# Queries without zero blocks: score and state products of 48 rows, two heads on two row tiles

## The chip, the cores and the metric

The kernel runs on one core of one Trainium2 chip. The metric is the device time of one execution in microseconds; the median of the runs counts. All arithmetic that matters here is float32.

## What is computed

Three layers in a row: a linear-attention recurrence, a soft mixture of experts, and an MLP with a squared ReLU. Only the first is touched. For 4 images (batch), 8 heads, 768 tokens and head size 48:

```python
for t in range(S):
    kt, vt, rt = (k[:, :, t], v[:, :, t], r[:, :, t])
    cur = np.einsum('bhd,bhe->bhde', u[None] * kt, vt)
    y[:, :, t] = np.einsum('bhd,bhde->bhe', rt, state + cur)
    state = w[None, :, :, None] * state + np.einsum('bhd,bhe->bhde', kt, vt)
```

`_moe_ref` then mixes the 3072 tokens of width 384 into 32 slots, sends each slot through one of 8 experts and mixes back, and `_moe2_ref` is `relu(x @ w_in)**2 @ w_out`.

## The kernel before, in words

The recurrence is done in six chunks of 128 tokens, and each chunk in four head pairs: 24 units, numbered n = 4 c + hp. A unit covers all four images b and both heads of its pair. The two heads stand on partitions 0 to 47 and 64 to 111 (`HEAD_ROWS`; `PAIR` is 112 partitions).

Each engine has its own program, in an order written by hand, and semaphores tie them together. One unit takes:

- SyncE (`load_unit`, line 314): loads `rk` (r and k with tokens last), once the queries of two units before are done, then `rkv` (r, k and v with tokens first) and a piece of the experts' weights.
- VectorE (`chunk`, in this order): `scale` multiplies k and r by powers of the decay, into `keys` (line 638) and `queries` (line 644). Then it waits for the diagonal of the unit before (`diag_done`). `advance` updates the state of two units before (line 680; in the first chunk a copy, line 676). `mask_scores` (line 667) copies the previous unit's scores from PSUM over the diagonal, where the mask says so. `sum_bonus` (line 662) sums `ruk`; `scale_n` (line 653) makes `keys_n`.
- GpSimd: `products` makes `ruk` = r u k in two steps (lines 402 and 405); `diagonal` (line 413) writes the bonus on the diagonal of `scores`, zero elsewhere, for the unit before. GpSimd runs one unit ahead with `ruk`.
- TensorE: `unit_scores` (line 865), then `unit_output` of the unit before, then `unit_state` (line 904).
- ScalarE copies the output and the state's increment out of PSUM.

`queries` has a block of zeros for each head: of an image's 256 columns the first 128 hold head 0 on partitions 0 to 47 with zeros below, the other 128 hold head 1 on partitions 64 to 111 with zeros above. One matmul of 112 rows and 256 columns then gives both heads' scores without mixing them, and the state product (line 887) of one head may take all 112 rows of the pair's state. GpSimd clears the four `queries` buffers once, at the start (line 395); VectorE fills the two blocks with one product each.

`unit_output` writes `y_ps`, one PSUM bank: for each image, two state products (not in the first chunk), then two products of masked scores and values (line 890), head 0 to partitions 0 to 47, head 1 to partitions 64 to 111. So they all work on two column tiles, with 112 or 128 rows.

The second unit of every chunk but the first (and the end) also brings the previous chunk's output into token order and forms its logits: `pair_logits` (line 839), a group of transposes (`turn_x`, line 847) after each image's scores, and `token_logits` (line 854). That is done between the unit's scores and the output of the unit before.

After the last unit come the experts and the MLP, whose weights are loaded as the recurrence frees their room.

Of the kernel before, what the change touches and what calls it, by code (L numbers as in the profile page):

```python
# [54 lines left out]
def program(nc, rk_t, rkv_n, w_t, u, phi, w1, w2, w_in, w_out, out):  # L55
# [32 lines left out]
    queries = [place(f"queries{i}", [P, B, 2, P]) for i in range(4)]  # L88
# [3 lines left out]
    scores = [place(f"scores{i}", [P, B, 2, P]) for i in range(2)]  # L92
# [5 lines left out]
    bonus = [place(f"bonus{i}", [P, B, 2]) for i in range(2)]  # L98
# [17 lines left out]
    assert place.end <= loads_end and queries_at == room_at + 4 * KD * FE and 4 * KE * DM <= 4 * (HP - 1) * B * 2 * P  # L116
# [49 lines left out]
    with stack:  # L166
# [30 lines left out]
        q_cleared = sem("q_cleared")  # L197
# [179 lines left out]
        def _(pool):  # L377
# [16 lines left out]
            for i in range(HP):  # L394
                nc.gpsimd.memset(queries[i][:, :, :, :], 0.0).then_inc(q_cleared, 1)
# [13 lines left out]
            def diagonal(m, hp):  # L409
# [4 lines left out]
                    scores[hp % 2][:, :, :, :].rearrange("p b h t -> p (b h) t"),  # L414
                    ident[:, :].unsqueeze(1).broadcast_to([P, 2 * B, P]),
                    bonus[hp % 2][:, :, :].rearrange("p b h -> p (b h)").unsqueeze(2).broadcast_to([P, 2 * B, P]),
# [175 lines left out]
        def _(ve):  # L592
# [40 lines left out]
            def scale(c, hp):  # L633
# [7 lines left out]
                if isinstance(c, int) and c == 0:  # L641
                    ve.wait_ge(q_cleared, hp + 1)
                for half, rows in enumerate(HEAD_ROWS):
                    last = nc.vector.tensor_tensor(queries[hp][rows, :, half], rk[hp % 2][rows, 0],  # L644
                                                   q_pow[rows, hp].unsqueeze(1).broadcast_to([D, B, P]), ALU.mult)
                last.then_inc(qk_done, 1)
# [10 lines left out]
            def sum_bonus(c, hp):  # L657
# [4 lines left out]
                nc.vector.reduce_sum(bonus[hp % 2][:, :, :], ruk[hp % 2][:, :, :].rearrange("p b (h d) -> p b h d", d=D),  # L662
                                     AX.X).then_inc(bonus_done, 1)

            def mask_scores(hp):

                nc.vector.copy_predicated(scores[hp % 2][:, :, :, :].rearrange("p b h t -> p (b h) t"),  # L667
# [165 lines left out]
        def _(pe):  # L833
# [24 lines left out]
            def unit_scores(c, hp, with_x):  # L858
# [5 lines left out]
                for b in range(B):  # L864
                    last = nc.tensor.matmul(score_ps[hp % 2][:, 2 * P * b:2 * P * (b + 1)], keys[hp % 2][0:PAIR, b],  # L865
                                            queries[hp][0:PAIR, b].rearrange("p h t -> p (h t)"), start=True, stop=True)
# [9 lines left out]
            def unit_output(m, c, hp):  # L876
# [6 lines left out]
                for b in range(B):  # L883
                    cols = slice(P * b, P * (b + 1))
                    if carried:
                        for half in range(2):
# [38 lines left out]
            chunk(0, True)  # L925
            pe.wait_ge(params_in, 3 * 16)
            pe.wait_ge(const_step, FOLD)
            chunk(1, False)
            with pe.Fori(2, CH) as c:
                chunk(c, False)  # L930

# [217 lines left out]
```

## Time and profile before

| | us |
|---|---|
| median of 3 runs | 467.32 |
| lowest, highest | 465.28, 467.35 |
| span of the profiled execution, first to last instruction | 464.3 |
| busy in it: TensorE, VectorE, ScalarE, GpSimd | 405.0, 331.9, 174.4, 153.1 |

No time of the profiled execution other than its span is shown; the median is 3.0 us above the span. The busy times are over the whole span, in which the recurrence is the first 176 us or so and the MLP the last 230. The page's chain of waits has 43% of the span in the MLP's output matmuls, which the change does not touch, and for the recurrence the diagonal on GpSimd (8%), the mask (4%) and the queries (4%). A row of the timeline merges neighbours of one line and operation ("x8"); in brackets stand the engine's idle time before it and what ended it. A float32 matmul leaves two records, so eight records are four matmuls.

### The profile page before, as it was taken

The page shows a single profiled execution, that of the slowest core. Times are in us where ns is not written, and L with a number is a line of the kernel's source. Part 1 is how long each engine was busy: PE and PEld are TensorE (multiplying, and loading weights), DVE is VectorE, ACT ScalarE, POOL GpSimd, SP SyncE. Part 2 cuts the span into 40 slices and gives each one's busy share as a digit, 9 for nine tenths or more (in the row PEclk, how much of TensorE's full clock was granted, in tenths as well). Part 3 has the DMA queues.
Part 4 walks back from the last instruction along what each step waited for, and adds up shares of the span by engine and source line. Part 5 has one row for each costly group of instructions (what it writes and reads, how often), then busy time and mean ns, then how long its engine had stood idle before and what let it go on. Part 6 is the DMA issues. An engine that isn't in the chain of part 4 may idle for free.

```text
span 464.3 us, 8783 instructions
## 1 busy us (share of the span) xinstructions
PE 405.0 (87%) x3096; PEld 349.0 (75%) x3096; DVE 331.9 (71%) x439; ACT 174.4 (38%) x312; POOL 153.1 (33%) x111
## 2 busy tenths in 40 slices
PE   0856968778787889999679999999999999999997
PEld 0544857657676766235279999999999999999997
DVE  8599999999999994611596565565556556556553
ACT  2011313123031314012535555555555555555552
POOL 6578878898888850110550000000000000000000
PEclk9957999999998989899889999999999999999999
DMA  6966667667666769999600010001001001001001
GB/s 174 243 195 193 202 206 218 183 201 231 194 196 203 225 238 316 373 373 403 212 0 1 1 68 2 1 1 68 0 0 68 0 0 68 0 0 68 1 0 68
DMA packets 31844, 60.30 MB, mean 130 GB/s; under 512 B 2640, under 2 KB 25296, under 8 KB 31440
## 3 DMA queue, kind: packets, MB, share of 16 engines
q1 hardware_dynamic: 31824, 60.02, 40.9%
q8 instruction: 13, 0.21, 0.2%
q14 instruction: 7, 0.06, 0.1%
HBM read 55.30 MB, written 4.72 MB: 129 GB/s over the span
## 4 chain that ended last, share of the span: by engine, by line
PE 61%; DVE 14%; POOL 10%; issue 5%; DVEq 1%; ACT 1%; POOLq 0%; ACTq 0%
PE out_ps L1081 43%; POOL scores L413 8%; PE h_ps L1059 5%; DVE scores L667 4%; DVE queries L644 4%; PE wide L997 3%; PE wide L1022 2%; PE score_ps L865 2%; DVE bonus L662 1%; DVE state L680 1%; PE y_ps L890 1%; POOL ruk L402 1%; POOL ruk L405 1%; PE wide L948 1%; DVE keys L638 1%
## 5 line engine op out<-in xcount | busy, mean ns | idle before, releaser
L1081 PE MATMUL out_ps<-w_hi,act_hi 128*128 128x384 f32 x384 | 130.5, 340 | 5.2 <-DVE act_lo L819 4.0
L1081 PE MATMUL out_ps<-w_hi,act_lo 128*128 128x384 f32 x384 | 131.0, 341 | 0.0
L1081 PE MATMUL out_ps<-w_lo,act_hi 128*128 128x384 f32 x384 | 130.5, 340 | 0.0
L814 DVE TENSOR_TENSOR act<-relu_h 128x512 f32<-128x512 f32 x96 | 68.2, 711 | 78.3 <-ACT relu_h L576 78.3
L576 ACT ACTIVATE relu_h<-h_ps 128x512 f32<-128x512 f32 x96 | 57.3, 597 | 100.6 <-PE h_ps L1059 97.9
L865 PE MATMUL score_ps<-queries,keys 112*128 112x256 f32 x192 | 60.5, 454 | 29.7 <-DVE queries L644 29.7
L413 POOL TENSOR_TENSOR scores<-ident,bonus 128x1024 f32<-128x1024 f32 x24 | 74.4, 3101 | 23.2 <-DVE bonus L662 23.2
L1081 PEld LDWEIGHTS out_ps<-w_hi,act_hi 128*128 128x128 f32 x384 | 72.7, 189 | 6.2 <-ACT act_hi L579 3.3
L1081 PEld LDWEIGHTS out_ps<-w_lo,act_hi 128*128 128x128 f32 x384 | 72.9, 190 | 3.8
L1081 PEld LDWEIGHTS out_ps<-w_hi,act_lo 128*128 128x128 f32 x384 | 72.5, 189 | 0.0
L819 DVE TENSOR_TENSOR act_lo<-act,act_hi 128x512 fp32r<-128x512 f32 x96 | 68.4, 713 | 4.6 <-ACT act_hi L579 1.0
L865 PEld LDWEIGHTS score_ps<-queries,keys 112*128 112x128 f32 x192 | 39.3, 222 | 41.8 <-DVE queries L644 24.1
L644 DVE TENSOR_TENSOR queries<-rk,q_pow 48x512 f32<-48x512 f32 x48 | 67.4, 1405 | 0.3
L579 ACT ACTIVATE act_hi<-relu_h 128x512 fp32r<-128x512 f32 x96 | 60.9, 634 | 3.9
L474 ACT ACTIVATE x_t<-y_ps 112x512 f32<-112x512 f32 x24 | 14.3, 597 | 111.2 <-PE y_ps L890 111.2
L890 PE MATMUL y_ps<-scores,rkv 128*48 128x128 f32 x384 | 38.0, 286 | 1.8 <-DVE scores L667 1.8
L1059 PE MATMUL h_ps<-mix_t,gin 128*128 (+1 forms) x96 | 38.0, 398 | 0.0
L887 PE MATMUL y_ps<-queries,state 112*48 112x128 f32 x320 | 32.6, 278 | 4.3 <-DVE scores L667 4.1
L667 DVE COPY_PREDICATED scores<-mask,score_ps 128x1024 f32<-128x1024 uint32 x24 | 32.0, 1333 | 4.8 <-POOL scores L413 4.8
L402 POOL TENSOR_TENSOR ruk<-rkv 128x384 f32<-128x384 f32 x24 | 31.0, 1291 | 10.8 <-DMA rkv<-in_rkv_n 8.5
L890 PEld LDWEIGHTS y_ps<-scores,rkv 128*48 128x48 f32 x384 | 24.6, 129 | 4.3 <-DVE scores L667 2.9
L887 PEld LDWEIGHTS y_ps<-queries,state 112*48 112x48 f32 x320 | 18.6, 123 | 10.8 <-issue 7.5
(145 smaller groups left out, 369.1 us busy)
## 6 DMA issues: line engine op xcount, KB each, us to landing
rkv<-in_rkv_n SPq DMA_DIRECT2D x24, 576.0 KB, 4.6
rk<-in_rk_t SPq DMA_DIRECT2D x48, 192.0 KB, 3.2
w_sb<-in_w SPq DMA_DIRECT2D x24, 384.0 KB, 5.1
w_room<-in_w SPq DMA_DIRECT2D x4, 1536.0 KB, 11.1
out_dram<-y_sb SPq DMA_DIRECT2D x5, 768.0 KB, 3.5
w_x<-in_w SPq DMA_DIRECT2D x2, 1536.0 KB, 14.0
w_w<-in_w SPq DMA_DIRECT2D x4, 768.0 KB, 11.5
w_in_sb<-in_w_in SPq DMA_DIRECT2D x3, 1024.0 KB, 13.0
```

The costliest lines, as they stand in the source:

```text
L413: nc.gpsimd.tensor_tensor(scores[hp % 2][:, :, :, :].rearrange("p b h t -> p (b h) t"), ident[:, :].unsqueeze(1).broadcast_to([P, 2 * B, P ...
L576: nc.scalar.activation(relu_h[f % 2][:, :], h_ps[f % 4][:, :], ACT.Relu).then_inc(relu_done, 1)
L579: nc.scalar.activation(act_hi[f % 4][:, :], relu_h[f % 2][:, :], ACT.Square).then_inc(act_hi_done, 1)
L644: last = nc.vector.tensor_tensor(queries[hp][rows, :, half], rk[hp % 2][rows, 0], q_pow[rows, hp].unsqueeze(1).broadcast_to([D, B, P]), AL ...
L667: nc.vector.copy_predicated(scores[hp % 2][:, :, :, :].rearrange("p b h t -> p (b h) t"), mask[:, :].unsqueeze(1).broadcast_to([P, 2 * B, P]),
L814: nc.vector.tensor_tensor(act[f % 2][:, :], relu_h[f % 2][:, :], relu_h[f % 2][:, :], ALU.mult).then_inc(act_done, 1)
L819: nc.vector.tensor_tensor(act_lo[f % 4][:, :], act[f % 2][:, :], act_hi[f % 4][:, :].bitcast(F32), ALU.subtract).then_inc(act_lo_done, 1)
L865: last = nc.tensor.matmul(score_ps[hp % 2][:, 2 * P * b:2 * P * (b + 1)], keys[hp % 2][0:PAIR, b], queries[hp][0:PAIR, b].rearrange("p h t ...
L887: nc.tensor.matmul(y_ps[SECOND * half:SECOND * half + D, cols], state[0:PAIR, hp, b], queries[hp][0:PAIR, b, half], start=True, stop=False)
L890: last = nc.tensor.matmul(y_ps[SECOND * half:SECOND * half + D, cols], rkv[hp][:, 2, b, D * half:D * (half + 1)], scores[hp % 2][:, b, hal ...
L1059: nc.tensor.matmul(h_ps[f % 4][:, :], gin[:, P * f:P * (f + 1)], mix_t[:, bass.ds(g * B, B), :], start=True, stop=True).then_inc(h_mm, 1)
L1081: last = nc.tensor.matmul(out_ps[t][:, 0:DM], a[f % 4][:, tok], w[:, f], start=(f == 0 and i == 0), stop=(f == NF - 1 and i == 2))
```

## The change

`queries` becomes one block: 112 partitions, 4 images, 128 tokens, and VectorE fills it with one product. GpSimd's clearing and its semaphore go. The scores of an image become two matmuls of 48 rows and 128 columns, one for each head: head 0 on rows 0 to 47, head 1 on rows 64 to 111, each into a PSUM bank of its own. The state products take the 48 rows of their head. `scores` and `bonus` are laid out by head first. TensorE's loop over the chunks is written out. Buffers elsewhere stay where they are (a gap of 8 KB a partition keeps them there).

```diff
@@ -85,17 +85,18 @@
-    queries = [place(f"queries{i}", [P, B, 2, P]) for i in range(4)]
+    cursor[0] += 4 * (KE * DM - 2 * B * P)
+    queries = [place(f"queries{i}", [P, B, P]) for i in range(4)]
...
-    scores = [place(f"scores{i}", [P, B, 2, P]) for i in range(2)]
+    scores = [place(f"scores{i}", [P, 2, B, P]) for i in range(2)]
...
-    bonus = [place(f"bonus{i}", [P, B, 2]) for i in range(2)]
+    bonus = [place(f"bonus{i}", [P, 2, B]) for i in range(2)]
...
@@ -391,8 +391,6 @@
-            for i in range(HP):
-                nc.gpsimd.memset(queries[i][:, :, :, :], 0.0).then_inc(q_cleared, 1)
...
@@ -638,12 +636,9 @@
                 wait(ve, y_done, n - 3)
-                if isinstance(c, int) and c == 0:
-                    ve.wait_ge(q_cleared, hp + 1)
-                for half, rows in enumerate(HEAD_ROWS):
-                    last = nc.vector.tensor_tensor(queries[hp][rows, :, half], rk[hp % 2][rows, 0],
-                                                   q_pow[rows, hp].unsqueeze(1).broadcast_to([D, B, P]), ALU.mult)
-                last.then_inc(qk_done, 1)
+                nc.vector.tensor_tensor(queries[hp][0:PAIR], rk[hp % 2][0:PAIR, 0],
+                                        q_pow[0:PAIR, hp].unsqueeze(1).broadcast_to([PAIR, B, P]),
+                                        ALU.mult).then_inc(qk_done, 1)
...
@@ -862,8 +857,10 @@
                 for b in range(B):
-                    last = nc.tensor.matmul(score_ps[hp % 2][:, 2 * P * b:2 * P * (b + 1)], keys[hp % 2][0:PAIR, b],
-                                            queries[hp][0:PAIR, b].rearrange("p h t -> p (h t)"), start=True, stop=True)
+                    for half, rows in enumerate(HEAD_ROWS):
+                        at = BANK * half + P * b
+                        last = nc.tensor.matmul(score_ps[hp % 2][:, at:at + P], keys[hp % 2][rows, b],
+                                                queries[hp][rows, b], start=True, stop=True)
...
@@ -883,13 +880,13 @@
                     if carried:
-                        for half in range(2):
-                            nc.tensor.matmul(y_ps[SECOND * half:SECOND * half + D, cols], state[0:PAIR, hp, b],
-                                             queries[hp][0:PAIR, b, half], start=True, stop=False)
+                        for rows in HEAD_ROWS:
+                            nc.tensor.matmul(y_ps[rows, cols], state[rows, hp, b], queries[hp][rows, b],
+                                             start=True, stop=False)
                     for half in range(2):
                         last = nc.tensor.matmul(y_ps[SECOND * half:SECOND * half + D, cols],
                                                 rkv[hp][:, 2, b, D * half:D * (half + 1)],
-                                                scores[hp % 2][:, b, half], start=not carried, stop=True)
+                                                scores[hp % 2][:, half, b], start=not carried, stop=True)
...
@@ -925,8 +922,7 @@
-            chunk(1, False)
-            with pe.Fori(2, CH) as c:
+            for c in range(1, CH):
                 chunk(c, False)
```

On VectorE, one unit of the second chunk, in program order (names are buffers, numbers their copies). Before:

```order
L638 TENSOR_TENSOR keys_58<-rk_56,k_pow 112x512
L644 TENSOR_TENSOR queries_62<-rk_56,q_pow 48x4x128 x2
L680 SCALAR_TENSOR_TENSOR state<-state,w_88,state_in_74 112x192
L667 COPY_PREDICATED scores_73<-mask,score_ps 128x1024
L662 TENSOR_REDUCE bonus_79<-ruk_68 128x8
L653 TENSOR_TENSOR keys_n_70<-rkv_66,kn_pow 128x384
```

Now:

```order
L636 TENSOR_TENSOR keys_58<-rk_56,k_pow 112x512
L639 TENSOR_TENSOR queries_62<-rk_56,q_pow 112x512
L675 SCALAR_TENSOR_TENSOR state<-state,w_88,state_in_74 112x192
L662 COPY_PREDICATED scores_73<-mask,score_ps 128x1024
L657 TENSOR_REDUCE bonus_79<-ruk_68 128x4x2
L648 TENSOR_TENSOR keys_n_70<-rkv_66,kn_pow 128x384
```

One queries product stands where two stood; the order of the rest is the same.

On TensorE, the unit that also turns the previous chunk's output, from its pair logits into the output of the unit before. Before:

```order
L839 MATMUL lg_ps<-x_t,phi_sb 32x512 x4
L865 MATMUL score_ps<-queries_61,keys_59 128x256
L847 MATMUL x_ps<-ident,x_t 128x112 x4
L865 MATMUL score_ps<-queries_61,keys_59 128x256
L847 MATMUL aux_ps<-ident,x_t 128x112 x4
L865 MATMUL score_ps<-queries_61,keys_59 128x256
L847 MATMUL x_ps<-ident,x_t 128x112 x4
L865 MATMUL score_ps<-queries_61,keys_59 128x256
L847 MATMUL aux_ps<-ident,x_t 128x112 x4
L854 MATMUL lg_ps<-fold_50,logits_t 128x128 x4
L887 MATMUL y_ps<-queries_60,state 48x128 x2
L890 MATMUL y_ps<-scores_72,rkv_64 48x128 x2
```

Now:

```order
L834 MATMUL lg_ps<-x_t,phi_sb 32x512 x4
L862 MATMUL score_ps<-queries_61,keys_59 128x128 x2
L842 MATMUL x_ps<-ident,x_t 128x112 x4
L862 MATMUL score_ps<-queries_61,keys_59 128x128 x2
L842 MATMUL aux_ps<-ident,x_t 128x112 x4
L862 MATMUL score_ps<-queries_61,keys_59 128x128 x2
L842 MATMUL x_ps<-ident,x_t 128x112 x4
L862 MATMUL score_ps<-queries_61,keys_59 128x128 x2
L842 MATMUL aux_ps<-ident,x_t 128x112 x4
L849 MATMUL lg_ps<-fold_50,logits_t 128x128 x4
L884 MATMUL y_ps<-queries_60,state 48x128 x2
L887 MATMUL y_ps<-scores_72,rkv_64 48x128 x2
```

Each image's scores are two matmuls of 128 columns in place of one of 256; nothing changed places. The state and output pairs of line 887 and 890 (now 884 and 887) alternate through all four images, as before.

## Rows read from the trace of the kernel before

**Rows 1.** The page's forty equal slices of the span: busy tenths.
```profile
DVE  8599999999999994611596565565556556556553
```

**Rows 2.** Views of source lines 644 and 413: duration ns min/median/max, first and last start.
```profile
L644 DVE TENSOR_TENSOR queries<-rk,q_pow x48: 672/692/2374, 10.2 to 169.3; 48x512 f32<-48x512 f32 x48
...
L413 POOL TENSOR_TENSOR scores<-ident,bonus x24: 1894/3333/3352, 18.7 to 172.2; 128x1024 f32<-128x1024 f32 x24
```

**Rows 3.** Timeline of one unit: start us, us, engine, line, operation, operands, count.
```profile
105.21 0.55 DVE L662 TENSOR_REDUCE bonus<-ruk 128x8 f32<-128x384 f32 x1
...
105.66 0.56 DVE L653 TENSOR_TENSOR keys_n<-rkv,kn_pow 128x384 f32<-128x384 f32 x1
...
105.83 3.33 POOL L413 TENSOR_TENSOR scores<-ident,bonus 128x1024 f32<-128x1024 f32 x1 [0.92 <-DVE bonus L662]
...
106.13 0.69 DVE L638 TENSOR_TENSOR keys<-rk,k_pow 112x512 f32<-112x512 f32 x1
...
106.73 2.98 DVE L644 TENSOR_TENSOR queries<-rk,q_pow 48x512 f32<-48x512 f32 x2
...
109.46 1.11 POOL L402 TENSOR_TENSOR ruk<-rkv 128x384 f32<-128x384 f32 x1 [0.30 <-DMA rkv<-in_rkv_n]
...
109.74 1.04 DVE L680 SCALAR_TENSOR_TENSOR state<-state,w,state_in 112x192 f32<-112x192 f32 x1
...
110.71 1.33 DVE L667 COPY_PREDICATED scores<-mask,score_ps 128x1024 f32<-128x1024 uint32 x1
...
111.93 0.54 DVE L662 TENSOR_REDUCE bonus<-ruk 128x8 f32<-128x384 f32 x1
```

**Rows 4.** Timeline of GpSimd, 10 to 180 us: the third and the twenty-third of 24 diagonals.
```profile
31.52 3.33 POOL L413 TENSOR_TENSOR scores<-ident,bonus 128x1024 f32<-128x1024 f32 x1 [1.87 <-DVE bonus L662]
...
165.95 2.21 POOL L413 TENSOR_TENSOR scores<-ident,bonus 128x1024 f32<-128x1024 f32 x1
```

**Rows 5.** Timeline of TensorE in a heavy unit; lastly the whole kernel's row of line 854.
```profile
98.80 0.43 PE L887 MATMUL y_ps<-queries,state 112*48 112x128 f32 x4 [0.44 <-DVE scores L667]
...
101.45 1.06 PE L839 MATMUL lg_ps<-x_t,phi_sb 112*32 112x512 f32 x8 [0.33 <-ACT x_t L474]
...
103.02 0.70 PE L865 MATMUL score_ps<-queries,keys 112*128 112x256 f32 x2 [0.50 <-DVE queries L644]
...
106.43 1.07 PE L854 MATMUL lg_ps<-fold,logits_t 128*128 128x128 f32 x8
...
107.43 0.43 PE L887 MATMUL y_ps<-queries,state 112*48 112x128 f32 x4
...
107.69 0.39 PE L890 MATMUL y_ps<-scores,rkv 128*48 128x128 f32 x4
...
109.01 0.39 PE L890 MATMUL y_ps<-scores,rkv 128*48 128x128 f32 x4
...
L854 PE MATMUL lg_ps<-fold,logits_t 128*128 128x128 f32 x48 | 6.4, 277 | 0.0
```

**Rows 6.** Timeline of VectorE near the end: a state update that waits for nothing.
```profile
163.63 0.42 DVE L680 SCALAR_TENSOR_TENSOR state<-state,w,state_in 112x192 f32<-112x192 f32 x1
```

**Rows 7.** Timeline of the recurrence's start, on GpSimd and VectorE.
```profile
11.30 1.15 POOL L402 TENSOR_TENSOR ruk<-rkv 128x384 f32<-128x384 f32 x1 [2.27 <-DMA phi_sb<-in_phi]
...
25.00 3.78 DVE L644 TENSOR_TENSOR queries<-rk,q_pow 48x512 f32<-48x512 f32 x2
...
27.24 0.99 POOL L402 TENSOR_TENSOR ruk<-rkv 128x384 f32<-128x384 f32 x1 [0.41 <-DMA rkv<-in_rkv_n]
```

**Rows 8.** Stretches (busy by engine, granted clock, DMA); scores at either clock.
```profile
24.50:31.52 7.02, 2.68 (x6) 2.19 (x7) 6.98 (x7) 0.30 (x1) 4.66 (x5) 0.50 0.55 152
...
112.55:119.37 6.82, 4.48 (x64) 3.80 (x61) 6.77 (x8) 0.82 (x2) 5.75 (x4) 1.00 0.68 201
...
28.84 3.78 PE L865 MATMUL score_ps<-queries,keys 112*128 112x256 f32 x8 [4.41 <-DVE queries L644]
...
109.77 1.99 PE L865 MATMUL score_ps<-queries,keys 112*128 112x256 f32 x8
```

More of the change, by code:

```diff
@@ L115, in program @@
     assert 2 * B * P == FE
-    assert place.end <= loads_end and queries_at == room_at + 4 * KD * FE and 4 * KE * DM <= 4 * (HP - 1) * B * 2 * P
+    assert place.end <= loads_end and queries_at == room_at + 4 * KD * FE
     experts_at = place.end
@@ L196, in program @@
         ps_cleared = sem("ps_cleared")
-        q_cleared = sem("q_cleared")
         const_step = sem("const_step")
@@ L413, in diagonal @@
                 nc.gpsimd.tensor_tensor(
-                    scores[hp % 2][:, :, :, :].rearrange("p b h t -> p (b h) t"),
+                    scores[hp % 2][:, :, :, :].rearrange("p h b t -> p (h b) t"),
                     ident[:, :].unsqueeze(1).broadcast_to([P, 2 * B, P]),
-                    bonus[hp % 2][:, :, :].rearrange("p b h -> p (b h)").unsqueeze(2).broadcast_to([P, 2 * B, P]),
+                    bonus[hp % 2][:, :, :].rearrange("p h b -> p (h b)").unsqueeze(2).broadcast_to([P, 2 * B, P]),
                     ALU.mult).then_inc(diag_done, 1)
@@ L661, in sum_bonus @@
                 wait(ve, diag_done, n - 1)
-                nc.vector.reduce_sum(bonus[hp % 2][:, :, :], ruk[hp % 2][:, :, :].rearrange("p b (h d) -> p b h d", d=D),
+                nc.vector.reduce_sum(bonus[hp % 2][:, :, :].rearrange("p h b -> p b h"), ruk[hp % 2][:, :, :].rearrange("p b (h d) -> p b h d", d=D),
                                      AX.X).then_inc(bonus_done, 1)
             def mask_scores(hp):
-                nc.vector.copy_predicated(scores[hp % 2][:, :, :, :].rearrange("p b h t -> p (b h) t"),
+                nc.vector.copy_predicated(scores[hp % 2][:, :, :, :].rearrange("p h b t -> p (h b) t"),
                                           mask[:, :].unsqueeze(1).broadcast_to([P, 2 * B, P]),
```

## The prediction

> **What bounds the kernel now.** The forty slices of the page come first: VectorE is at nine tenths through the first fifteen slices, the recurrence, and only there [rows 1]. The change touches nothing behind it except through the moment at which the recurrence ends. Next, the summary of single source lines: a queries product takes 0.67 us at least and 2.37 at most, the diagonal product on GpSimd 1.89 at least and mostly 3.33 [rows 2]. Two engines that at times stretch each other. The timeline of one unit shows how [rows 3]. The diagonal starts at 105.83 but ends 1.44 us later than an undisturbed one would, and it gets going just where the first queries product ends (106.73 + 0.67 = 107.40; 107.40 to its end 109.16 is 1.76). The pair of queries products takes 2.98: the second half runs only when the diagonal has ended, and ends 0.55 behind it, at 109.71. Then the first `ruk` product takes its turn (until 110.57, 0.86 behind 109.71), and the state update waits for that, 1.04 us where an undisturbed one took 0.42 [rows 6]. So products with two operands in SBUF take turns with GpSimd's, one at a time, and VectorE is never idle. One unit, bonus to bonus, is 111.93 - 105.21 = 6.72 us, and the twenty units between two diagonals far apart average (165.95 - 31.52) / 20 = 6.72 [rows 4]. The last view is TensorE's timeline in the one unit of four that also turns the previous chunk's output (I call it heavy) [rows 5].
>
> **The base.** The profiled execution spans 464.3 us; the median of the three times is 467.3, so 3.0 lie around the span or between executions. The change is summed on the profiled execution and applied to the median.
>
> **VectorE's edit.** One of two queries products goes; the one left has 112 partitions and as many elements in each, like the keys product, which takes 0.69 [rows 3], so the width is free. What that is worth is not 24 times the mean of 1.4, most of which is waiting. In the unit of rows 3 the order before the diagonal stays: bonus, keys_n, keys, one queries product, 2.19 us from the bonus's start; then the diagonal's 1.76. Behind it stood the second queries product for 0.55. Now nothing stands there, and the next to ask is the `ruk` product, which GpSimd starts as soon as the diagonal ends; the state update cannot start sooner than 0.58 us behind it (109.74 - 109.16). So `ruk` goes first: about 0.09 to begin (its undisturbed 0.99 [rows 7] less the 0.86, less the little by which it overlaps the diagonal's end), 0.86, then 0.22 of the state update (its end 110.78 less 110.57), then 1.15 to the next bonus. Sum: 2.19 + 1.76 + 0.09 + 0.86 + 0.22 + 1.15 = 6.27; gain 0.45 a unit, **9.0 us over twenty units**. The ends: nothing, if the freed turn is only waited out elsewhere; 1.0 a unit if the state update slips in ahead of `ruk`. I take 0.45, from the order in which rows 3 show the starts. At the beginning, the unit at 25.00 has both queries products blocked, 3.78 in all, one by the diagonal and one by a `ruk` [rows 7]: between 0.7 and 1.4 less, I take 1.0. The four memsets are worth nothing: GpSimd waits 2.27 us for a DMA before its first product anyway [rows 7]. The layouts of `scores` and `bonus` keep their elements: nothing. On SyncE the loads that wait for the queries go out some 2.3 us sooner, past nothing else; that helps no one, since the next keys come a unit later.
>
> **TensorE's edit, plain part.** The scores of one image were one product of 256 columns; now two of 128 columns on two row tiles. No row here has two row tiles. The nearest are two column tiles, the pairs of the output: between 107.69 and 109.01 six groups of four records take 0.22 each, 0.055 a record, where records of 128 columns on the whole array come every (1.07 - 0.28) / 7 = 0.113 [rows 5]. So pairs on column tiles overlap. If row tiles do too, the scores of a unit lose 4 x 0.22 = 0.9 us; if not, nothing. I take 0.9. The state products were already pairs on column tiles, and stay 0.22 an image.
>
> Writing out the loop over the chunks removes a branch at the first unit of a chunk, a light one, where TensorE has idle time to hide it, and adds instructions to fetch: nothing both ways; in the heavy unit, without that cover, neither falls.
>
> **TensorE's edit, the switches.** The state products now use 64 rows and 48 columns, the output products beside them all 128 rows, and they alternate image by image: seven changes of tile shape inside each unit's output. Rows 5 show what a change of shape (there, of the columns alone) costs: after eight records from 106.43 the next should start at 107.34, and starts at 107.43; the next group follows after 0.26 in place of 0.22. Together 0.13. So the output of a unit grows by 7 x 0.13 = 0.9. In the heavy unit the scores (64 rows) alternate with the turned output (128 rows, 128 columns of weights): seven more, each about 0.10 plus one record's 0.11 for weights that can no longer be loaded ahead, an estimate from the same rows, 0.21: 1.5. The ends are nothing (shapes that differ in rows alone need no pause) and twice this.
>
> **Does that reach the end?** In a light unit no: its TensorE work is 4.48 of 6.82 us [rows 8], it loses 0.9 and gains 0.9. In the heavy unit, yes. From the start of one unit's output (98.80) to the end of the next one's (109.01 + 0.39 = 109.40) TensorE needs 10.6, and the state update that waits for it starts at 109.74: 0.34 to spare. After: 10.6 + 0.9 + 0.9 (two outputs) + 1.5 - 0.9 (scores) - 0.5 (the wait for queries between 102.51 and 103.02, which come sooner) = 12.5. Allowed were 10.94; two shorter periods take 0.9, the mask that opens the first output comes 0.46 sooner behind the diagonal, and the update may start some 0.15 later before it delays anything: 10.65. **Late by 1.85, five times, 9.2 us.** The last output of all has no other work beside it, and adds 0.9.
>
> **Sum.** -9.0 - 1.0 + 9.2 + 0.9 = +0.1: VectorE's gain is given back on TensorE. Forecast 467, no change that can be told (under 0.5%, 2.3 us).
>
> **Rivals.**
> *No pause between row shapes.* TensorE then needs 10.6 - 0.9 - 0.5 = 9.2 of 10.65 and never binds: -9.0 - 1.0, 457. For it: what rows 5 show are changes of columns. Against: the pause there is the same kind of event, and the rows of the array are in use in both shapes.
> The Trainium skill, "TensorEngine Tiling (Array Packing)", Overview, says that changing the tiling mode drains the engine, rows or columns alike, without a price; by it, the forecast's side of this question is the right one.
>
> *The two heads' state products do not overlap.* Both write `y_ps`, one PSUM bank, from two row tiles, where today two column tiles write it. Taken one after the other they add 4 x 0.22 = 0.9 to each unit's output, 1.8 to the heavy chain, 9 us in five, 0.9 at the tail: 477, slower. It decides from the point at which a pair costs 0.06 more than now. Nothing in the profile speaks for or against row tiles sharing a bank; for column tiles they overlap.
> The Trainium skill, same page, Restrictions and Gotchas, says that row tiles cannot access one PSUM bank at the same time; by it the time would be this rival's. No run here shows it yet.
>
> *TensorE's clock.* In the stretch 24.50 to 31.52 the granted clock is 0.50 (1.2 GHz), and the scores take 3.78 for eight records, 1.99 at 1.00 [rows 8]. A light unit after the change has fewer columns to stream. At 1.2 GHz its 4.5 us would be some 8.5, 2 us over the period: two such units are felt, five make 477. Against: the light unit of rows 8 is granted 1.00 though it idles a third of the time.
>
> *The port goes strictly to who asked first.* The diagonal, started during keys_n, would then run ahead of keys and queries, and the `ruk` products would fall between these; the state update would come last: bonus 0.45, keys_n 0.55, diagonal 1.76, then keys, `ruk`, queries, `ruk` (2 x 0.55 + 2 x 0.86), 0.22, 1.15, 6.95 a unit, 472. Rows 3 speak against it: keys and the first queries product went ahead of a waiting diagonal.
> The Trainium skill, "SBUF — State Buffer", Who interferes with whom, has the pair of ports as an exclusive lock for whoever issues first; the trace agrees on the lock (0.67 against 2.37), not on the order.
>
> *The state update ahead of `ruk`*, and no pause on TensorE: 5.7 a unit, 446.
>
> **Chances.** Forecast (both halves nearly cancel, 463 to 471) 0.37; no pause 0.25; no overlap 0.15; clock 0.12; state ahead 0.05; first asked 0.04; something else 0.02. Of the forecast's 0.37 I count 0.24 within 0.5%, the rest half to each side. Faster: 0.25 + 0.05 + 0.07 = 0.37; slower: 0.15 + 0.12 + 0.03 + 0.06 + 0.01 = 0.37; same 0.26. The range 455 to 478 takes in the first four cases with their ends; the likeliest alone would be 463 to 471.
>
> **What would show it.** Right: light units of about 6.27 from diagonal to diagonal, the unit after a heavy one near 8.1; queries a single row of 0.7; `ruk` directly behind the diagonal and the state update at 1 us or more; output records with a gap of about 0.13 at each state-to-output change; the idle time before the state update put down to TensorE's `y_ps`. Wrong: the unit after a heavy one no longer than the others (no pause); state records in pairs 0.1 apart rather than together (no overlap); a granted clock of 0.50 inside the recurrence beyond its first 50 us; a diagonal of 1.9 to 2.4 with keys behind it (order of the port).

## The result and the profile after

The changed kernel takes 480.22 us in the median of four executions (476.86 to 492.12), the kernel before 466.43 beside it: a ratio of **1.027, 95% interval 1.020 to 1.033, slower**. The forecast was no change, 467, in a range of 455 to 478: wrong, and outside the range. (Ratios here leave out executions over 1.5% above the fastest of their kernel, medians and profiles don't: where a kernel's times scatter, the two differ by up to 1%.)

The page of the changed kernel first: VectorE's slices, then TensorE's granted clock by slice.
```profile
DVE  7586564654636517370198556556556556556553
PEclk9996958869659569999978999999999999999999
```
The same row of the kernel before:
```profile
PEclk9957999999998989899889999999999999999999
```
VectorE, at nine tenths before [rows 1], is at three to eight, mostly four to six: it no longer bounds the recurrence. Between the fourth and the fifteenth slice TensorE's clock, at eight tenths and more from the fifth slice on before, dips to five and six tenths again and again.

The profiled execution spans 480.3, 16.0 more than before. The third diagonal starts at 29.26 and the twenty-third at 182.22 (31.52 and 165.95 before [rows 4]): the start gains 2.3, the twenty units lose 18.5 (152.96 against 134.43), the unit behind them gains 0.7, and all that follows loses 0.4. So the question is about the twenty units alone. Stretches of the changed kernel, each from one diagonal to the next (length, busy us of PE, PEld, DVE, ACT, POOL, granted clock, DMA share, GB/s):
```profile
85.33:91.67 6.34, 4.42 (x68) 2.87 (x68) 4.50 (x7) 0.82 (x2) 5.29 (x3) 1.00 0.82 259
91.67:97.90 6.23, 6.23 (x60) 4.12 (x56) 3.72 (x7) 0.93 (x2) 5.23 (x4) 0.51 0.64 180
97.90:105.34 7.44, 7.38 (x60) 3.02 (x56) 3.77 (x7) 0.93 (x2) 5.29 (x4) 0.50 0.65 192
105.34:115.53 10.19, 9.68 (x114) 6.79 (x112) 3.77 (x7) 3.67 (x8) 5.30 (x4) 0.99 0.47 146
115.53:121.89 6.36, 4.43 (x68) 2.87 (x68) 4.51 (x7) 0.82 (x2) 5.29 (x4) 1.00 0.81 248
121.89:128.10 6.21, 6.21 (x62) 4.16 (x60) 4.05 (x7) 0.93 (x2) 5.22 (x4) 0.55 0.66 202
128.10:135.43 7.33, 7.27 (x58) 2.94 (x56) 4.00 (x7) 0.93 (x2) 5.29 (x3) 0.50 0.58 177
135.43:148.77 13.34, 12.81 (x110) 9.24 (x112) 3.78 (x7) 3.65 (x8) 5.30 (x4) 0.71 0.32 92
```
A pattern of four: a light unit at full clock (6.34 and 6.36; 6.27 was forecast), one of the same length near half clock (1.2 GHz), one of 7.3 to 7.4 at half clock, in which TensorE is busy nearly throughout, and the stretch of the heavy unit (the heavy stretch from here on), 10.2 or 13.3. The five heavy stretches are 7.34, 9.22, 10.19, 13.34 and 13.55 long. At 13.34 TensorE is busy for 12.81 at a mean clock of 0.71.

Who waits for it shows in the summary of VectorE's lines, the state update of the changed kernel over the twenty units (17 records; in the first chunk it is a copy, on another line):
```profile
L675 DVE SCALAR_TENSOR_TENSOR state<-state,w,state_in 112x192 f32<-112x192 f32 x17 | 12.8, 750 | 64.7 <-PE y_ps L887 55.2 <-POOL scores L411 9.5
```
and of the kernel before:
```profile
L680 DVE SCALAR_TENSOR_TENSOR state<-state,w,state_in 112x192 f32<-112x192 f32 x17 | 16.6, 977 | 1.4 <-PE y_ps L890 0.9
```
VectorE idles 55.2 us for TensorE's output where it idled 0.9.

The timeline of TensorE in the changed kernel has an output at full clock, and the scores alternating with the turned output at half clock:
```profile
110.20 0.42 PE L884 MATMUL y_ps<-queries,state 48*48 48x128 f32 x4
110.55 0.43 PE L887 MATMUL y_ps<-scores,rkv 128*48 128x128 f32 x4
110.91 0.42 PE L884 MATMUL y_ps<-queries,state 48*48 48x128 f32 x4
...
135.33 0.80 PE L862 MATMUL score_ps<-queries,keys 48*128 48x128 f32 x4
136.06 1.00 PE L842 MATMUL x_ps<-ident,x_t 112*128 112x112 f32 x4
137.00 0.80 PE L862 MATMUL score_ps<-queries,keys 48*128 48x128 f32 x4
...
146.62 1.16 PE L862 MATMUL score_ps<-queries,keys 48*128 48x128 f32 x16
```
Groups of four records, state and output by turns, come every 0.355 us where they came every 0.22 [rows 5]: 0.135 for each change of shape. The scores of a whole unit take 1.16 at full clock, 1.99 before [rows 8]: two row tiles do run side by side (here each writes its own PSUM bank). An image of the heavy unit takes 1.67 at half clock (137.00 - 135.33).

VectorE and GpSimd in a light unit of the changed kernel, by the timeline:
```profile
115.53 3.35 POOL L411 TENSOR_TENSOR scores<-ident,bonus 128x1024 f32<-128x1024 f32 x1 [4.81 <-DVE bonus L657]
118.83 0.99 POOL L400 TENSOR_TENSOR ruk<-rkv 128x384 f32<-128x384 f32 x1
...
116.43 0.69 DVE L639 TENSOR_TENSOR queries<-rk,q_pow 112x512 f32<-112x512 f32 x1
...
118.96 1.08 DVE L675 SCALAR_TENSOR_TENSOR state<-state,w,state_in 112x192 f32<-112x192 f32 x1 [1.85 <-POOL scores L411]
```
One queries product of 0.69, the diagonal ending 1.76 behind it, then `ruk`, then the state update: the order and lengths that the prediction worked out of [rows 3].

### The profile page after: what moved, and what is told of

Its sections match the earlier page's. It is cut to its first block, busy times and chain, and to the rows that moved or that the text cites. A ratio compares the mean times of both kernels' runs of the same rounds, so it can differ in the third digit from the quotient of the medians.

```text
span 480.3 us, 9086 instructions
## 1 busy us (share of the span) xinstructions
PE 432.5 (90%) x3288; PEld 347.6 (72%) x3288; DVE 276.4 (58%) x415; ACT 175.6 (37%) x312; POOL 144.2 (30%) x107
## 4 chain that ended last, share of the span: by engine, by line
PE 71%; POOL 5%; issue 5%; DVE 4%; DMA 3%; ACT 1%; SPq 1%; DVEq 1%; POOLq 0%; ACTq 0%
PE out_ps L1077 43%; PE y_ps L884 5%; PE y_ps L887 5%; POOL scores L411 5%; PE h_ps L1055 5%; PE score_ps L862 3%; DMA w_w<-in_w 3%; DVE scores L662 2%; PE lg_ps L834 2%; PE x_ps L842 1%; PE aux_ps L842 1%; PE lg_ps L849 1%; PE wide L993 1%; SPq L355 1%; PE wide L944 1%
## 5 line engine op out<-in xcount | busy, mean ns | idle before, releaser
L1077 PE MATMUL out_ps<-w_hi,act_hi 128*128 128x384 f32 x384 | 131.9, 343 | 4.0 <-DVE act_lo L814 2.4
L411 POOL TENSOR_TENSOR scores<-ident,bonus 128x1024 f32<-128x1024 f32 x24 | 76.2, 3176 | 48.9 <-DVE bonus L657 48.9
L887 PE MATMUL y_ps<-scores,rkv 128*48 128x128 f32 x384 | 48.2, 352 | 8.6 <-DVE scores L662 8.4
L884 PE MATMUL y_ps<-queries,state 48*48 48x128 f32 x320 | 40.2, 335 | 12.5 <-DVE scores L662 12.5
L675 DVE SCALAR_TENSOR_TENSOR state<-state,w,state_in 112x192 f32<-112x192 f32 x18 | 13.2, 732 | 66.6 <-PE y_ps L887 55.2
L862 PE MATMUL score_ps<-queries,keys 48*128 48x128 f32 x384 | 41.7, 358 | 3.8 <-DVE queries L639 3.8
L862 PEld LDWEIGHTS score_ps<-queries,keys 48*128 48x128 f32 x384 | 32.6, 243 | 15.6 <-issue 8.8
L887 PEld LDWEIGHTS y_ps<-scores,rkv 128*48 128x48 f32 x384 | 21.5, 147 | 29.1 <-issue 19.4
L884 PEld LDWEIGHTS y_ps<-queries,state 48*48 48x48 f32 x320 | 15.2, 135 | 30.7 <-DVE scores L662 15.2
L400 POOL TENSOR_TENSOR ruk<-rkv 128x384 f32<-128x384 f32 x24 | 24.0, 1000 | 7.3 <-DMA rkv<-in_rkv_n 4.9
```

The source lines that it names most:

```text
L400: nc.gpsimd.tensor_tensor(ruk[hp % 2][:, :, :], rkv[hp][:, 0], rkv[hp][:, 1], ALU.mult).then_inc(rk_prod_done, 1)
L411: nc.gpsimd.tensor_tensor(scores[hp % 2][:, :, :, :].rearrange("p h b t -> p (h b) t"), ident[:, :].unsqueeze(1).broadcast_to([P, 2 * B, P ...
L862: last = nc.tensor.matmul(score_ps[hp % 2][:, at:at + P], keys[hp % 2][rows, b], queries[hp][rows, b], start=True, stop=True)
L884: nc.tensor.matmul(y_ps[rows, cols], state[rows, hp, b], queries[hp][rows, b], start=True, stop=False)
L887: last = nc.tensor.matmul(y_ps[SECOND * half:SECOND * half + D, cols], rkv[hp][:, 2, b, D * half:D * (half + 1)], scores[hp % 2][:, half, ...
L1077: last = nc.tensor.matmul(out_ps[t][:, 0:DM], a[f % 4][:, tok], w[:, f], start=(f == 0 and i == 0), stop=(f == NF - 1 and i == 2))
```

## The experiments

Two theories. *Pauses*: the changes of tile shape make TensorE's chain around the heavy unit too long. *Clock*: with the shorter scores TensorE's clock falls, and that alone decides. The runs are called e1 to e13. All ratios are against the kernel before, run on the same chip.

### Fewer changes of shape

e1, the scores of the heavy unit ahead of all transposes:
```diff
-                    if b == B - 1:
-                        last.then_inc(score_done, 1)
-                    if with_x:
+                last.then_inc(score_done, 1)
+                if with_x:
+                    for b in range(B):
```


> The changed kernel with one thing else: in the heavy unit the eight scores products stand together ahead of the transposes, so that 7 of the 8 changes of tile shape there go. Theory 1 (the pauses at shape changes make TensorE's chain in the heavy unit too long, and the lateness is multiplied where its granted clock falls): each pause with the weights not loaded ahead is about 0.12 us (0.955 against 0.83 an image), 4 images, 0.5 to 1.5 us a heavy unit, five units, partly at half clock: 3 to 9 us less than the changed kernel, 472 to 477. Theory 2 (the granted clock alone decides, pauses are a side matter): 478 to 482, and the clock still 0.50 in the third unit of a chunk. Against both: the state update's first transposes come later in this order, which may cost the 1 us that the scores now stand in front of them; then 480 to 484.

Measured: 484.94, ratio 1.039 (1.033 to 1.045). Both theories missed the time, and the third range, 480 to 484, missed it by a little. The clock was at 0.50 to 0.56 in the third units, as the second theory has it, and at 0.69 to 0.78 in four of five heavy stretches, where the change had two such. What makes it slower than the change stays open.

e2, the state product second and first by turns:
```diff
+                    state_first = b % 2 == 1
+                    if carried and state_first:
+                        from_state()
                     for half in range(2):
                         last = nc.tensor.matmul(y_ps[SECOND * half:SECOND * half + D, cols],
...
+                    if carried and not state_first:
+                        last = from_state()
```


> The changed kernel with one thing else: in every unit's output the state product comes second and first by turns (output, state, state, output, output, state, state, output), so 4 changes of tile shape in place of 7. Theory 1: 3 pauses of 0.135 us less, 0.4 us in each of two outputs of the chain over a heavy unit, 0.8 by five, 4 us, up to 6 where the clock is at half: 474 to 476. Theory 2: less time in the output but the same columns, so the clock does as before: 478 to 481.

Measured: 470.38 in the median of ten executions from 464.51 to 480.34, ratio 1.003 (0.999 to 1.007): 10 us less than the change, more than pauses at full clock explain. Its output has eight state records in a row:
```profile
112.29 0.64 PE L886 MATMUL y_ps<-queries,state 48*48 48x128 f32 x8
112.86 0.64 PE L893 MATMUL y_ps<-scores,rkv 128*48 128x128 f32 x8
```
Four records and a change of shape took 0.355; eight take 0.57, so the second four add 0.22, as pairs on column tiles do. One after the other they would add four times 0.113 [rows 5], 0.45. The two heads' state products, on two row tiles, overlap in one PSUM bank.

e3, both:

> The changed kernel with both orders at once (scores together in the heavy unit, state products second and first by turns). Theory 1: the gains add up, 2.0 to 2.7 us a heavy unit and five of them, 10 to 14 us: 466 to 470, the unit after a heavy one 7 to 8 us where the clock is full. Theory 2: 478 to 482, or no better than the better of the two alone, with units of 10 to 13 us at a clock of 0.7 as they are now.

Measured: 466.03, ratio 0.996 (0.992 to 1.000). Its stretches:
```profile
75.29:82.06 6.77, 5.82 (x84) 4.52 (x84) 4.20 (x7) 1.97 (x5) 5.34 (x3) 1.00 0.89 249
...
94.60:100.93 6.33, 6.27 (x61) 3.75 (x60) 3.80 (x7) 1.22 (x3) 5.32 (x4) 0.58 0.73 211
100.93:109.57 8.64, 7.87 (x108) 6.25 (x106) 3.73 (x7) 3.15 (x8) 5.29 (x3) 1.00 0.51 173
```
The heavy stretch is 6.77 where the clock ahead of it was full, 8.64 behind a unit at 0.58: the clock matters. That the pauses do too is seen against e4, below: 7.87 with all of them, at full clock.

### The clock by itself

e4, the light units' scores done twice:
```diff
-                    for half, rows in enumerate(HEAD_ROWS):
+                    for half, rows in list(enumerate(HEAD_ROWS)) * (1 if with_x else 2):
```


> The changed kernel with the scores products of the three light units of a chunk done twice (the second time into the same place): TensorE has 1.16 us more to do in a unit, about as much as before the change, while the heavy units are as changed. Theory 2 (the clock falls because light units keep TensorE less busy): the granted clock stays at 1.00 in the recurrence, the slow heavy units of 13 us go, and the time falls to 467 to 473 in spite of the added work. Theory 1: the added work lies in light units with idle time; 480 to 484 and a clock that falls as before.

Measured: 466.80, ratio 0.999 (0.995 to 1.003): *more* work on TensorE took 13 us off the changed kernel, pauses unchanged. The mean granted clock of the profiled execution is 0.982, the change's 0.908. Its stretches, and of the last one the start of the output ahead of the heavy unit's scores and the end of the one behind them:
```profile
96.09:102.38 6.29, 6.24 (x62) 3.07 (x62) 4.45 (x7) 1.52 (x3) 5.31 (x3) 0.73 0.76 231
102.38:111.44 9.06, 9.06 (x117) 6.82 (x116) 3.78 (x7) 3.06 (x7) 5.29 (x3) 1.00 0.48 145
...
117.81:123.99 6.18, 5.16 (x82) 3.64 (x80) 4.08 (x7) 0.82 (x2) 5.22 (x3) 1.00 0.59 172
123.99:130.31 6.32, 5.98 (x72) 3.38 (x72) 4.47 (x7) 1.98 (x5) 5.32 (x3) 1.00 0.88 272
130.31:138.18 7.87, 7.87 (x107) 5.90 (x106) 3.77 (x7) 2.50 (x6) 5.30 (x3) 1.00 0.48 137
```
```profile
123.53 0.42 PE L884 MATMUL y_ps<-queries,state 48*48 48x128 f32 x4 [1.02 <-DVE scores L662]
135.33 0.43 PE L887 MATMUL y_ps<-scores,rkv 128*48 128x128 f32 x4
```
Where the clock is full, light units are 6.2 to 6.4, the heavy stretch is 7.87, and TensorE's chain around the heavy unit takes 12.2 us (123.53 to 135.76): the forecast's picture (6.27, 8.1 and 12.5), and the forecast's time, 467. One light unit at 0.73 makes the next heavy stretch 9.06. The five heavy stretches (7.43, 7.85, 9.06, 7.87, 9.03) are 9.9 over five of 6.27, where the forecast has 9.2. That the two sums meet so closely is in part luck: two of the five come behind a unit at 0.73, and the first, one of whose two outputs has no state products, is shorter.

### VectorE's edit and the pauses, each alone

e5, in the kernel before, one queries product:
```diff
-                for half, rows in enumerate(HEAD_ROWS):
+                for half, rows in list(enumerate(HEAD_ROWS))[:1]:
```


> The kernel before with the first of its two queries products alone: the second head's block of the queries stays zero, so the second head's scores and state products are left out of the result, while TensorE's instructions, shapes and columns are those of before. Theory (VectorE's share of the change is worth 0.45 us a unit and some 2 us at the start, and is lost on TensorE alone): units of 6.27 us, heavy ones 6.3 to 6.7, the granted clock as before, 454 to 458. Rival (TensorE binds the unit of before as closely as VectorE, so that there was nothing to gain): 464 to 467.

Measured: 456.94, ratio 0.980 (0.976 to 0.983). Two of its stretches, the first the heavy one:
```profile
97.33:103.63 6.30, 6.11 (x78) 5.32 (x78) 4.20 (x7) 2.02 (x5) 5.31 (x3) 1.00 0.73 222
103.63:109.97 6.34, 4.41 (x64) 3.79 (x61) 4.49 (x7) 0.82 (x2) 5.28 (x3) 1.00 0.76 219
```
The twenty units (28.66 to 153.86) average 6.26. VectorE's gain is real, and TensorE as it was allowed it.

e6, the changed kernel with two queries products of 48 partitions:
```diff
-                nc.vector.tensor_tensor(queries[hp][0:PAIR], rk[hp % 2][0:PAIR, 0],
...
+                for rows in HEAD_ROWS:
+                    last = nc.vector.tensor_tensor(queries[hp][rows], rk[hp % 2][rows, 0],
```


> The changed kernel with VectorE's edit undone in time: the queries product in two halves of 48 partitions, as before, TensorE as changed. Theory (light units are bound by VectorE, the unit behind a heavy one by TensorE): 15 light units 0.45 us longer and the start 1 to 2 us later, 8 to 9 us over the changed kernel, 487 to 489. Rival (TensorE's row tiles bind every unit, VectorE's gain is already worth nothing): 480 to 482. A clock that falls less because the chain is slower elsewhere would show as a mean granted clock above 0.93.

Measured: 490.72 in the median of four executions from 483.33 to 496.84, too scattered for a ratio, and the median is nearer the theory's 487 to 489 than the rival's. The one profile is of the lowest, 483.33, near the rival's 480 to 482:
```profile
104.10:110.92 6.82, 6.76 (x54) 2.78 (x52) 6.07 (x8) 0.93 (x2) 5.76 (x4) 0.50 0.70 203
110.92:121.32 10.40, 9.90 (x114) 7.00 (x112) 6.04 (x8) 3.66 (x8) 5.74 (x4) 0.97 0.54 166
```
In it light units are longer again (6.6 to 6.8, two of 7.6 and 7.9), yet the twenty (30.81 to 182.78) take 151.97, not more than the changed kernel's 152.96: while TensorE is late, VectorE's 0.45 a unit is worth nothing there. Whether that holds for the two executions of 496 and 497 is not shown. And the clock falls as in the change (0.50 above) with VectorE back at its old length, so the shorter unit was not what pulled it down.

e7, in the kernel before, the state products alone on row tiles:
```diff
-                            nc.tensor.matmul(y_ps[SECOND * half:SECOND * half + D, cols], state[0:PAIR, hp, b],
-                                             queries[hp][0:PAIR, b, half], start=True, stop=False)
+                            nc.tensor.matmul(y_ps[rows, cols], state[rows, hp, b],
+                                             queries[hp][rows, b, half], start=True, stop=False)
...
-            chunk(1, False)
-            with pe.Fori(2, CH) as c:
+            for c in range(1, CH):
```


> The kernel before with the state products alone on two row tiles (48 rows each, 7 changes of tile shape in an output), the scores and both queries products as before, TensorE's loop over the chunks written out as in the change. Theory 1 (a change costs 0.135 us at full clock): 0.95 us more in each of the two outputs of a heavy chain that has 0.34 to spare, so the unit behind a heavy one 7.4 to 8.2 us and the others 6.72; five times 0.7 to 1.5 and 0.9 at the end: 470 to 475, the granted clock as before. Theory 2 (without the shorter scores the clock holds and the pauses alone cost nothing): 465 to 468.

Measured: 472.78, ratio 1.010 (1.006 to 1.015). A light and a heavy stretch:
```profile
92.90:99.53 6.63, 5.16 (x58) 3.21 (x56) 6.58 (x8) 0.82 (x2) 5.29 (x3) 1.00 0.79 217
...
106.39:114.16 7.77, 7.34 (x77) 5.03 (x77) 6.80 (x8) 2.08 (x5) 5.74 (x3) 1.00 0.80 220
```
Pauses alone cost 1.0 us a heavy stretch (7.77 against 6.72) and leave the clock full nearly everywhere. The written-out loop costs nothing that shows in light units: they are 6.4 to 6.9, but for one of 7.76, in which the diagonal ran ahead of the keys (2.14 long, the keys 2.38).

### Both remedies, and a version without the output's pauses

e8, both orders of e3, and from the second chunk on the light units' scores twice:
```diff
+                    for half, rows in list(enumerate(HEAD_ROWS)) * (1 if with_x or c == 0 else 2):
```


> The changed kernel with both orders of the third experiment and, from the second chunk on, the scores products of the light units done twice. If the two causes (pauses in the heavy chain, the granted clock) are all that the change lost: the clock at 1.00, light units of 6.3 us and the unit after a heavy one 6.5 to 7.0, as it was there at full clock; 15 x 6.3 + 5 x 6.8 = 128.5 for twenty units against 134.4 before, and some 2 us at the start: 457 to 460, faster than both kernels. Rival (a third bound, such as the transfers): no better than the third experiment, 463 to 467.

Measured: 463.06, ratio 0.990 (0.986 to 0.994): better than e3, short of the theory's 457 to 460. In the profiled execution (466.32, the slowest of six) the clock still fell to 0.51 and 0.53 in two light units (the heavy stretches behind them 9.0 and 9.1), and the other heavy stretches were 7.35 to 7.8; VectorE still waited 27.8 us for TensorE's output.

So e9 takes the output's pauses out altogether (those of the heavy unit's scores stay): ScalarE keeps a zero-padded copy of the state, which moves the zero blocks from the queries to where there is time. (The copy lies where an expert's first weights are loaded later; those now wait for the last output.)
```diff
+                        for half, rows in enumerate(HEAD_ROWS):
+                            last = nc.scalar.activation(state_z[rows, older[2], :, half], state[rows, older[2]], ACT.Copy)
+                        last.then_inc(z_done, 1)
...
-                    ve.wait_ge(y_done, m + 1)
-                    ve.wait_ge(state_done, m - HP + 1)
+                    ve.wait_ge(z_done, m - HP + 1)
...
-                        for rows in HEAD_ROWS:
-                            nc.tensor.matmul(y_ps[rows, cols], state[rows, hp, b], queries[hp][rows, b],
+                        for half in range(2):
+                            nc.tensor.matmul(y_ps[SECOND * half:SECOND * half + D, cols], state_z[0:PAIR, hp, b, half],
+                                             queries[hp][0:PAIR, b], start=True, stop=False)
```


> The changed kernel with the state products back on the whole array without zero blocks in the queries: ScalarE copies each updated state, one head beside the other, into a zero-padded copy that TensorE reads (two activations of 48 partitions a unit, three units before they are needed), so that an output has no change of tile shape and the state update no longer waits for TensorE's output. The scores stay on row tiles. If the pauses of the output are what lengthens the heavy chain at full clock: heavy units 6.3 to 7 where the clock is 1.00. Whether the clock falls is the question: if TensorE's shorter work alone pulls it down, it is at 0.50 in light units as in the changed kernel, and the time is 462 to 470; if the pauses pulled it down, the clock stays at 1.00 and the time is 455 to 459.

Measured: **457.19, ratio 0.979 (0.975 to 0.984): faster than both kernels.** Three of its stretches, the last the heavy one, and its output in TensorE's timeline:
```profile
85.52:91.72 6.20, 4.92 (x66) 4.63 (x64) 4.17 (x7) 1.65 (x4) 5.22 (x4) 0.72 0.76 235
91.72:98.03 6.31, 5.97 (x80) 4.22 (x76) 4.46 (x7) 3.17 (x8) 5.31 (x3) 1.00 0.75 217
98.03:104.32 6.29, 5.49 (x88) 5.00 (x88) 4.45 (x7) 2.75 (x7) 5.30 (x4) 1.00 0.61 182
```
```profile
99.90 0.39 PE L896 MATMUL y_ps<-scores,rkv 128*48 128x128 f32 x4
100.12 0.39 PE L893 MATMUL y_ps<-queries,state_z 112*48 112x128 f32 x4
100.34 0.39 PE L896 MATMUL y_ps<-scores,rkv 128*48 128x128 f32 x4
```
Groups every 0.22 again. The clock still falls (to 0.50 once in the first chunks, 0.59 to 0.81 in places later), less deeply than with the pauses, and does no harm: heavy stretches are 6.1 to 6.3.

The same with the light units' scores twice (e10), and with the heavy unit's scores grouped as well (e11):

> The ninth experiment with the scores products of the light units done twice from the second chunk on. If work on TensorE holds the clock: 1.00 in nearly all units, light units 6.27, heavy ones 6.3 to 7.0, 455 to 459, faster than both kernels. If the clock follows the pauses: as the ninth, or 1 to 2 us slower.

> The tenth with the scores of the heavy unit ahead of its transposes, 1 change of tile shape there in place of 7. If the pauses of the heavy unit's scores still bind: 1 to 4 us less than the tenth. If VectorE and GpSimd bind all units by then: the same within 1 us; if the transposes, later in this order, hold up the state that follows: 1 to 5 us more.

Measured: 457.66, ratio 0.979 (0.976 to 0.982), and 457.46, ratio 0.977 (0.973 to 0.982). With slack in TensorE's chain neither the clock nor the remaining pauses make a difference that shows.

e9 removed two things: the output's pauses, and the state update's wait for TensorE's output. One at a time, first the pauses without the wait (e12), then the wait without the pauses (e13):
```diff
+                        for half, rows in enumerate(HEAD_ROWS):
+                            nc.tensor.matmul(y_ps[rows, cols], state_z[rows, hp, b, half], queries[hp][rows, b],
```


> The ninth experiment with the state products on row tiles again (48 rows each, read from ScalarE's copy), so that the pauses of the changed kernel are back and only the wait of the state update for TensorE's output is gone. Theory A (the pauses lengthen the chain, whichever wait carries them to VectorE): the mask and the diagonal still wait for TensorE, heavy units of 9 us and more, the clock at 0.50 in places, 470 to 480. Theory B (the wait of the state update is what turns TensorE's lateness into time): 457 to 460, the clock falling without harm.


```diff
+                    ve.wait_ge(y_done, m + 1)
                     ve.wait_ge(z_done, m - HP + 1)
```


> The ninth experiment with the state update waiting for TensorE's output again, though it needs nothing from it, and the state products without pauses as there. Theory A (pauses): heavy units of at most 7 us at full clock, some late where the clock falls ahead of them, 457 to 463. Theory B (the wait): most of the loss comes back, 468 to 480.

Measured: pauses without the wait 468.62, ratio 0.998 (0.993 to 1.003); the wait without pauses 463.63 in the median of ten executions from 456.70 to 469.35, ratio 0.984 (0.979 to 0.989; 0.994 by the medians). Two stretches of each, of e12 first (the profile of e13 is of an execution of 464.40):
```profile
66.38:72.66 6.28, 6.22 (x54) 2.78 (x52) 4.43 (x7) 1.65 (x4) 5.29 (x3) 0.50 0.62 191
72.66:85.11 12.45, 12.45 (x92) 8.37 (x88) 5.34 (x9) 2.96 (x7) 5.30 (x4) 0.60 0.32 104
```
and of e13:
```profile
93.73:100.03 6.30, 6.24 (x61) 4.45 (x58) 4.45 (x7) 2.25 (x5) 5.30 (x4) 0.58 0.72 219
100.03:108.41 8.38, 7.86 (x107) 6.71 (x107) 3.77 (x7) 3.78 (x9) 5.30 (x4) 1.00 0.49 157
```
By the medians, each against the kernel before beside it, e9 brings back 23.3 us, taking out the wait alone 11.8, taking out the pauses alone 16.8: half and more each, together more than the whole, so the loss is not a sum of the two. With the pauses, a heavy stretch whose clock stays down (0.60) is 12.45 long even without the wait: there the state update waits 4.92 us and is released by TensorE's scores.

## Why the prediction was wrong

**VectorE's edit: right.** 6.27 a unit was forecast, 6.26 measured with TensorE's work as before, and 457.3 (467.3 - 10.0) against 456.94. The start gained more than the 1.0 taken (2.3 in the change, 2.9 in e5). Two readings were loose, without effect: VectorE is at nine tenths from the third slice on, not in the first two [rows 1], and the last piece of the state update is 0.21, not 0.22.

**The plain part and the switches: right.** Scores shorter by 0.83 (0.9 forecast); a pause of 0.135 (0.13 taken from a change of columns, [rows 5], and valid for rows). With the clock put back (e4) TensorE's chain around the heavy unit is 12.2, 12.5 forecast, the heavy stretch 7.87, 8.1 forecast, and the kernel 466.8, 467 forecast.

**The step that failed** is the term "late by 1.85, five times, 9.2 us", because it was worked out at full clock, and with it the "in a light unit no" ahead of it. The rival on TensorE's clock was set beside the term as another case (0.12), not on top of it. Measured, the five heavy stretches are 53.64 in all, 22.3 over five of 6.27: 13 us more than the term, where e4, with the clock nearly full, has 9.9. The other fifteen take 99.32, 5.3 over fifteen of 6.27, nearly all of it in five light units at about half clock (7.28 to 7.44). Start, last unit and tail came out 2.5 better than forecast; together that is the 16 us in span.

The rival's sign, a granted clock of 0.50 beyond the first 50 us, came. Its price, 477, was near by luck: it has five light units 2 us over their period, where those at half clock are 1.0 to 1.2 over, and nothing more for the heavy stretches, where most of the loss is. Its argument against itself ("granted 1.00 though it idles a third of the time") was a row of the kernel before, and did not carry over to other products. Nor is it a case beside the forecast's: a light unit that half the clock pushes beyond its period hands the heavy unit over late, sometimes still at half clock (the scores at 135.33), and there the pauses have already used up the 0.34 to spare.

**The other rivals.** *No pause* fell (0.355 against 0.22). *No overlap in one bank* fell (eight state records in 0.57, e2). The Trainium skill, "TensorEngine Tiling (Array Packing)", has the drain at a change of mode under Tiling Modes, Key Properties, not under the Overview that the prediction names; the trace agrees, with 0.135 us for each change. What the Trainium skill, same page, Restrictions and Gotchas, says of row tiles and one PSUM bank did not hold for two heads on different partitions of the bank; the measurement decides. *First asked* fell in the light unit of the changed kernel shown above: keys and queries ran ahead of a waiting diagonal. *State update ahead of `ruk`* did not occur in the light unit shown, but in some units of e9, where `ruk` waited for a transfer; one from 130.02 takes 5.59 (5.7 forecast). There the diagonal also ran ahead of the keys (2.21 long, the keys 2.38), so it is not the unit that the 5.7 was worked out for.

The chance given to "slower" was 0.37; it should have been higher: two causes were priced as if only one could come true, and here one fed the other.

## What to carry to other kernels

Where an edit makes an engine's work shorter, ask of that engine's clock what the edit does to it, and price every other term at both clocks: of the two causes here, the pauses of 0.135 us cost about 6 us alone in the kernel before (e7) and about 10 once VectorE's unit is shorter and the clock nearly full (e4 against e9), the falling clock nothing that shows where TensorE had slack (e9 against e10), and both together 23 us, the whole gain and 14 more. Zero padding that a bound engine writes can be moved to an engine with idle time instead of being taken out by smaller tiles; here ScalarE's copies kept VectorE's gain of 2% and TensorE's tile shape. And doing useless work twice is a cheap experiment that tells a clock from a pause.

## What was not expected of the hardware

The clock fell where TensorE's busy share had not. The light stretch 115.53 to 121.89 of the changed kernel is busy for 4.43 of 6.36 us (70%) and the next is granted 0.55; before, one is busy for 4.48 of 6.82 (66%) [rows 8] and the clock stays at 1.00. Nor did TensorE stand still for longer: its longest wait in that stretch of the changed kernel is 1.93 us, and in the kernel before one of 2.16 is followed by a full clock (1.00 from 99.07 to 105.83). The two rows, of the changed kernel first:
```profile
121.35 0.42 PE L884 MATMUL y_ps<-queries,state 48*48 48x128 f32 x4 [1.93 <-DVE scores L662]
...
96.37 1.99 PE L865 MATMUL score_ps<-queries,keys 112*128 112x256 f32 x8 [2.16 <-DVE queries L644]
```
What differs in TensorE's light units is the form of the work: scores as pairs of 48 rows in 1.16 us, not one of 112 rows in 1.99, and state products of 48 rows with pauses. With the long scores kept, the same pauses left the clock at 1.00 in nearly all units (e7); with the short scores done twice it was 1.00 or 0.73 in the last three chunks (e4); with short scores and no pauses in the output it fell in part (e9). More than this the runs don't tell: what brings the clock down stays open.
